# Two expert layers behind windowed attention: the output sums turned by VectorE in 32x32 blocks and stored in runs of 128 bytes, in place of TensorE's transposes

## What is computed

```python
w = softmax(weight_gen)                  # (2, 4096, 8 heads, 7 taps)
x = einsum('bshk,bskhg->bshg', w, x_unf) # 7 earlier tokens, 192 = 8 heads x 24
h = x @ w_in                             # 8192 x 192 by 192 x 2048
g = h * np.cos(h);  x = g @ w_out        # back to 192
h = x @ moe2_w_in
g = np.maximum(0.01 * h, h);  out = g @ moe2_w_out   # (8192, 192), float32
```

## Time and profile before

| | |
|---|---|
| median of 3 runs | 1163.77 us (1163.77 to 1166.3) |
| profiled execution | 1166.25 us |
| its span, first to last instruction | 1164.4 us |
| TensorE (PE) busy | 1146.1 us, 98% |
| VectorE (DVE) busy | 900.9 us, 77% |
| ScalarE (ACT) busy | 735.9 us, 63% |
| granted TensorE clock, mean | 0.997 |

### The profile page before, as it was taken

The page is one execution under the profiler, slowest core; times in us unless marked ns, Lnnn a source line. Parts: engine busy times, 40 slices in busy tenths (PEclk is TensorE's granted clock), DMA queues, the critical chain, the costliest instruction groups (busy, mean ns, idle before and its releaser), DMA issues.

```text
span 1164.4 us, 23292 instructions
## 1 busy us (share of the span) xinstructions
PE 1146.1 (98%) x10170; PEld 950.1 (82%) x10170; DVE 900.9 (77%) x862; ACT 735.9 (63%) x804; POOL 84.9 (7%) x81
## 2 busy tenths in 40 slices
PE   7889999999999999999999999999999999999998
PEld 5768888888888888888888888888888888888876
DVE  8878797878879788697786868868697886968433
ACT  5666674766657676575755747566575655757554
POOL 5850000000000000000000000000000000000000
PEclk9999999999999999999999999999999999999999
DMA  9760101001010000101001010000101001000000
GB/s 260 202 120 1 35 1 49 1 2 49 1 49 1 20 30 1 49 1 49 1 2 48 1 48 1 22 28 1 48 2 49 1 1 48 1 15 1 15 1 28
DMA packets 20653, 37.40 MB, mean 32 GB/s; under 512 B 5196, under 2 KB 14794, under 8 KB 20168
## 3 DMA queue, kind: packets, MB, share of 16 engines
q1 hardware_dynamic: 16104, 30.66, 8.4%
q0 software_dynamic: 4448, 5.24, 2.5%
HBM read 29.61 MB, written 6.29 MB: 31 GB/s over the span
## 4 chain that ended last, share of the span: by engine, by line
PE 92%; DVE 2%; SPq 2%; POOL 2%; ACT 1%; issue 1%; DMA 1%; ACTq 0%; POOLq 0%
PE slot L1064 43%; PE acc_a L1064 28%; PE acc_b L1064 19%; DMA x_win<-in_x 1%; DVE g_lo L825 1%; POOL prods L307 1%; POOL prods L298 1%; SPq L463 0%; DVE prods L307 0%; POOL out_hi_lo L554 0%; PE slot L1009 0%; DVE gate L897 0%; PE acc_b L1037 0%; PE slot L996 0%; ACT g_hi L637 0%
## 5 line engine op out<-in xcount | busy, mean ns | idle before, releaser
L1064 PE MATMUL acc_a<-g_hi,out_hi_lo 64*128 64x512 f32 x2000 | 697.5, 389 | 0.0
L1064 PEld LDWEIGHTS acc_a<-g_hi,out_hi_lo 64*128 64x128 f32 x2000 | 369.0, 184 | 36.8
L825 DVE TENSOR_TENSOR g_lo<-gate,g_hi 128x1024 fp32r<-128x1024 f32 x248 | 303.6, 1224 | 117.5 <-ACT g_hi L637 116.9
L1064 PE MATMUL acc_b<-g_hi,out_hi_lo 64*128 64x512 f32 x1000 | 389.1, 389 | 1.6 <-DVE g_lo L825 1.5
L1064 PE MATMUL acc_b<-g_lo,out_hi_lo 64*128 64x512 f32 x1000 | 387.5, 387 | 0.0
L1064 PE MATMUL acc_a<-g_lo,out_hi_lo 64*128 64x512 f32 x1000 | 387.3, 387 | 0.0
L637 ACT ACTIVATE g_hi<-gate 128x1024 fp32r<-128x1024 f32 x248 | 262.9, 1060 | 94.3 <-PE acc_b L1064 77.5
L1064 PE MATMUL slot<-x_a_hi,in_a_lo 64*128 64x512 f32 x1024 | 299.6, 394 | 5.2 <-DVE g_lo L825 2.5
L1064 PE MATMUL slot<-x_b,in_b_hi 64*128 64x512 f32 x1024 | 296.4, 388 | 0.2 <-DVE x_b L839 0.2
L1064 PE MATMUL slot<-x_a_lo,in_a_hi 64*128 64x512 f32 x1024 | 296.3, 387 | 0.0
L1064 PE MATMUL slot<-x_a_hi,in_a_hi 64*128 64x512 f32 x1024 | 296.2, 387 | 0.0
(11 more groups left out here) (100 smaller groups left out, 1073.9 us busy)
## 6 DMA issues: line engine op xcount, KB each, us to landing
x_win<-in_x SPq DMA_DIRECT2D x14, 960.0 KB, 4.7
out<-result SPq DMA_DIRECT2D x16, 384.0 KB, 2.3
out_raw<-in_moe_w_out SPq DMA_DIRECT2D x3, 512.0 KB, 8.5
out_hi_lo<-in_moe_w_out POOLq DMA_DIRECT2D x2, 768.0 KB, 11.0
out_hi_lo<-in_moe_w_out POOLq DMA_DIRECT2D x1, 1536.0 KB, 14.5
taps_w<-in_weight_gen SPq DMA_DIRECT2D x2, 560.0 KB, 9.4
in_a_raw<-in_moe_w_in SPq DMA_DIRECT2D x1, 1024.0 KB, 5.3
out_raw<-in_moe_w_out SPq DMA_DIRECT2D x1, 1024.0 KB, 11.6
```

The lines of the kernel that those rows point to most:

```text
L825: nc.vector.tensor_tensor(g_lo[:, q % 2, :], result_of(i - b, q), g_hi[:, q % 2, :].bitcast(FP32), ALU.subtract)\
L1064: return nc.tensor.matmul(to, w[rows, :], x[rows, :], start=start, stop=stop)
```

## The change

The output step of the first 15 chunks goes. In its place DVE, at step 14 of iteration i, turns `res_a` and `res_b` of chunk i-2 in blocks of 32x32 (`turn_result`), after the low part of step 12's unit. Within such a block tokens and channels have then changed places, but the blocks stand where they stood, so the stores gather them: 24 DMAs a chunk, each with 32 partitions x 4 runs of 32 values (128 bytes). The last chunk goes through TensorE as before.

```diff
-OUTPUT_STEP = 13
+TURN_STEP = 14
+BLOCK = 32
...
-        if step == OUTPUT_STEP:
-            return "output" if 2 <= i <= LAST else None
...
+                to = out_rows[:, c * row:(c + 1) * row]\
+                    .rearrange("(k t) (j d) -> t j k d", t=BLOCK, j=J)
+                sp.wait_ge(turned, 2 * c + 1)
+                for j in range(J):
+                    for d in range(0, DA, BLOCK):
+                        sp.dma_start(to[:, j, :, d:d + BLOCK],
+                                     turned_a[d:d + BLOCK, j * P:(j + 1) * P]
+                                     .rearrange("t (k d) -> t k d", d=BLOCK)).then_inc(stored, 16)
+                sp.wait_ge(turned, 2 * c + 2)
...
+            def turn_result(i):
+
+
+                c = i - 2
+                if c:
+                    dve.wait_ge(stored, 16 * STORES * c)
+                dve.wait_ge(acc_a_out, second_phase(i - 1) + 1)
+                nc.vector.transpose(turned_a[:, :], res_a[:, :]).then_inc(turned, 1)
+                dve.wait_ge(acc_b_out, second_phase(i - 1) + 1)
+                nc.vector.transpose(turned_b[:, :], res_b[:, :]).then_inc(turned, 1)
...
+                if step == TURN_STEP and i >= 2:
+                    turn_result(i)
...
-                if after == OUTPUT_STEP and kind(i, after) == "output":
-                    both_products(i, q, i, q - LAG, lambda: wait_for_output(i))
-                    transpose_output(slots[OUTPUT_STEP % SLOTS])
```

More of the change, by code:

```diff
@@ L208, in window_attention_two_ffn @@
         result = sb("result", [P, J, dim])
+        turned_a = sb("turned_a", [P, N])
+        turned_b = sb("turned_b", [P, N // 2])
         ident = sb("ident", [P, P])
@@ L266, in window_attention_two_ffn @@
         acc_b_out = sem("acc_b_out")
+        turned = sem("turned")
         result_ready = sem("result_ready")
@@ L435, in result_of @@
             return gate[:, q % 2, :]
+        STORES = J * dim // BLOCK
         block = ctx.enter_context(nc.Block())
@@ L496, in store, with store_last @@
             def store(c):
-                sp.wait_ge(result_ready, c + 1)
-                sp.dma_start(out_rows[:, c * row:(c + 1) * row],
+                to = out_rows[:, c * row:(c + 1) * row]\
[7 more added lines that the diff above has]
+                sp.wait_ge(turned, 2 * c + 2)
+                for j in range(J):
+                    for d in range(0, DB, BLOCK):
+                        s = j // 2 * DB + d
+                        sp.dma_start(to[:, j, :, DA + d:DA + d + BLOCK],
+                                     turned_b[s:s + BLOCK, j % 2 * P:(j % 2 + 1) * P]
+                                     .rearrange("t (k d) -> t k d", d=BLOCK)).then_inc(stored, 16)
+            def store_last():
+                sp.wait_ge(result_ready, 1)
+                sp.dma_start(out_rows[:, (C - 1) * row:],
                              result[:, :, :].rearrange("p t d -> p (t d)")).then_inc(stored, 16)
@@ L509, in _ @@
                 load_x(i + 2)
-            for c in range(C - 4, C):
+            for c in range(C - 4, C - 1):
                 store(c)
-            sp.wait_ge(stored, 16 * C)
+            store_last()
+            sp.wait_ge(stored, 16 * (STORES * (C - 1) + 1))
         @block.gpsimd
@@ L659, in leave_mid_a, with leave_res_a @@
                 nc.scalar.activation(mid_a[:, :], acc_a[:, :], ACT.Copy).then_inc(acc_a_out, 1)
-            def leave_res_a():
+            def leave_res_a(i):
+                if i >= 2:
+                    act.wait_ge(turned, 2 * (i - 1) - 1)
                 nc.scalar.activation(
@@ L666, in leave_res_a, with move_result @@
                     .then_inc(acc_a_out, 1)
-            def move_result(i, step, c):
+            def move_result(i, step):
                 act.wait_ge(filled, fills(i, step))
-                if c >= 1:
-                    act.wait_ge(stored, c * 16)
                 src = slots[step % SLOTS]
@@ L718, in step_of @@
                     split_second_high(i, step)
-                if kind(i, step) == "output":
-                    move_result(i, step, i - 2)
                 if step == INPUT_STEP - 1 and input_splits(i, INPUT_STEP):
@@ L749, in step_of @@
                     act.wait_ge(summed, unit(i - 1, 15) + 1)
-                    leave_res_a()
+                    leave_res_a(i - 1)
                 first_read(i, step)
@@ L803, in _ @@
             act.wait_ge(summed, unit(LAST, 15) + 1)
-            leave_res_a()
-            move_result(LAST, FINAL_STEP, C - 1)
+            leave_res_a(LAST)
+            move_result(LAST, FINAL_STEP)
         @block.vector
@@ L1158, in wait_for_slot @@
                     pe.wait_ge(leaky_ready, second_units(j, UNITS.index(s)))
-                elif what == "input":
+                else:
                     pe.wait_ge(x1_ready, j * 2 + 4)
-                else:
-                    pe.wait_ge(result_ready, j - 1)
             def wait_to_fill(i, q):
@@ L1233, in wait_for_input @@
                 pe.wait_ge(att, i * ATT_STEPS + 2 * ATT_STEPS)
[L1235 to L1238, removed]
             def rest_of_iteration(i, q):
                 after = UNITS[q] + 1
-                if after == OUTPUT_STEP and kind(i, after) == "output":
-                    both_products(i, q, i, q - LAG, lambda: wait_for_output(i))
-                    transpose_output(slots[OUTPUT_STEP % SLOTS])
-                elif after == INPUT_STEP and kind(i, after) == "input":
+                if after == INPUT_STEP and kind(i, after) == "input":
                     both_products(i, q, i, q - LAG, lambda: wait_for_input(i, INPUT_STEP))
```

## The result

| | before | changed |
|---|---|---|
| median, 5 runs each on one chip | 1165.18 us (1163.77 to 1166.3) | 1158.62 us (1158.38 to 1160.24) |
| profiled execution | 1166.25 us | 1158.45 us |
| its span | 1164.4 us | 1156.7 us |

The ratio is 0.9948, 95% interval 0.9937 to 0.9960: 6.1 us faster, where 6.3 were forecast. The forecast time, 1157.5 us, was reckoned from 1163.77, the median of the first three runs of the kernel before; five runs give 1165.18. The measured 1158.62 lies in the range, 1155.0 to 1161.3.

A forecast was written before the change was run, and what follows sets the result against it. TensorE, busy for 98% of the span, was taken to bound the kernel. Its 6.6 us gained less 0.3 us lost to the turn gave -6.3 us, from 1163.77 to 1157.5 us, range 1155.0 to 1161.3.

The forecast's parts named there:

- TensorE's 0.44 us a chunk: TensorE, border of steps 12 and 14: removing the output step shortens 1.35 us to 0.91, 15 times, 6.6 us gained.
- ScalarE's moves 0: ScalarE, two moves a chunk removed: it is idle 26 us in 70, so this gives TensorE nothing, 0.
- The turn at 1.1 us: VectorE, step 14: both transposes together take 0.68 + 0.42 us, read from rows of the same shapes.
- turn in iterations 3 and 5, 0.3 us: VectorE ahead of the input split: 1.1 us of transposes exceed 0.93 us idle, so 0.3 us lost in all.
- grows from 0.3 to 0.5 us: Sign in iterations 3 and 5: TensorE's wait for step 14's low part lengthens by that much.
- SP at 0.45 us an issue, hidden: SP's queue: 24 stores take 10.8 us a chunk beside TensorE's work, and cost 0, at the end too.
- One store after the other: Rival: stores land singly, 2.3 us each, 55 us a chunk, delaying loads; about 1340 us. Chance 0.02.
- The window's load: Load behind the stores in SP's queue: lands at 639.1, VectorE reads at 663.36, 24 us to spare, cost 0.
- The covers of 2.5 and 0.9 us: VectorE time that transposes at step 14 may take for nothing: 2.5 us in iterations 2 and 4, 0.93 in 3 and 5.
- That of 5.1 us: Ordinary iterations: 3.50 us idle ahead of the input split plus 1.57 us slack hide transposes up to this length.

The follow-up runs named there:

- act_moves: The changed kernel with ScalarE's two moves a chunk put back at step 13, results unread; ratio to before 0.9950.
- no_turn: The changed kernel without VectorE's transposes and small stores, sums stored untransposed with two DMAs a chunk, so output order is wrong; ratio to before 0.9951.
- step8: The changed kernel with VectorE's transposes at step 8 in place of 14; ratio to before 0.9952.
- sine15: The changed kernel with ScalarE's sine table reload in iterations 1, 3 and 5 at step 15 in place of 14, behind the input split; ratio to before 0.9933.
- stores2: The changed kernel with each small store cut in two, 48 DMAs of 128 runs of 64 bytes a chunk; ratio to before 1.0011.
- turn3: The changed kernel with each of VectorE's transposes made three times, 3.4 us a turn; ratio to before 1.0012.

## Why the prediction was right

- **TensorE's 0.44 us a chunk are the gain: shown.** TensorE's transposes back, gain gone; ScalarE's moves back, gain kept. The distance of starts was the right measure: the busy times of the two groups of transposes, 0.41 + 0.29 us, would have promised 10.5 us.
- **ScalarE's moves 0: shown** by act_moves.
- **The turn at 1.1 us: right**, 0.70 + 0.41. The Trainium skill's table ("VectorE: DVE Perf Modes", "The three transpose paths"), scaled by blocks, gave 1.87 us. Its 311 ns are for one tile of 128x128 of two-byte values; between 128x256 and 128x512 here lie 302 ns for 256 columns, which leaves some 0.1 us fixed in each instruction, and six tiles count it six times. That accounts for a part of the difference only. The measurement decides.
- **The term "turn in iterations 3 and 5, 0.3 us": the step that failed.** It was worked out from 1.1 us of turn against 0.93 us of idle time ahead of the split, and the turn causes no loss there: it fits, no_turn and step8 have the same hole without it, and sine15 closes the hole with the turn in its place. The sum went wrong one step earlier. It gives TensorE its 0.44 us in all 15 iterations, though it says itself that in 3 and 5 TensorE already waits for step 14's low part. An engine that waits for another gains nothing by arriving earlier. So nearly the whole 0.44 us was lost, twice. Around iteration 3 it is 0.18 us ahead of the input step (the next point but one) and 0.23 us behind it, where the low part comes when ScalarE's table load lets it; around iteration 5 it is 0.18 and 0.25 us. That makes 0.8 us in place of 0.3. (The 0.3 us of the earlier trace rows were no measure of the wait: from start to start the old hole was 0.07 us over a border without one.)
- **The total came nearer than its terms, and that is luck.** 0.5 us more were lost than forecast, and 0.3 us came back with the hole of iteration 6, which nobody had seen. The sign that was to show the turn, a wait that "grows from 0.3 to 0.5 us", came true (0.30 to 0.51) for another reason.
- **A second, smaller hole** in iteration 3 (starts at 264.97, 265.23, 265.54, some 0.1 us) stands where TensorE waits for attention's last sum, over at 265.08; the later reload leaves it as it is. It goes with the 0.18 us that the period which ends there lacks. That cause is read from the timeline and wasn't tried.
- **SP at 0.45 us an issue, hidden: right**, 0.48, and stores2 showed where the cover ends. The Trainium skill's rule that runs under 512 bytes miss line rate and bring a read-modify-write ("DMA: Bandwidth & Descriptors", "Specifications") may hold of the engines' bandwidth, and no run here shows such an operation; but 128 bytes cost 11.5 ns a packet and the queue that issues was the limit. The rule had no say in the time.
- **One store after the other: excluded**; a store landed in 1.5 us in the median (3.7 at most), and 24 were issued in 11.5.
- **The window's load: right**, landed 27 us ahead of its use, where 24 were read off.
- **The covers of 2.5 and 0.9 us**: turn3 met them with 6.3 us, the clock left out, for 6.6. That of 5.1 us is shown up to 3.4.

## What to carry to other kernels

When one engine paces a loop, cost a change by the distance of starts on that engine across the place, with and without; busy times of overlapped instructions promise more. Work for another engine is free as long as it fits the idle time ahead of its next wait plus the slack of the one who waits for it; the same 3.4 us cost 7.4 us, or nothing that could be told, by their place. And a faster pacing engine uses up slack of its neighbours: look for the iterations in which it waits for them already. There count no gain at all, and look for what makes them late; moving it may bring the gain back.

## What the runs showed of the hardware

- A float32 transpose in 32x32 blocks on VectorE, 128x512, takes 0.70 us, 128x256 0.40; a subtraction of 128x512 takes 0.68.
- A store of 128 runs of 128 bytes from 32 partitions is issued in 0.43 us in the median and lands in 1.5; runs of 64 bytes don't change the 0.47 us from one issue to the next. The engines took 11.5 ns a packet of the 128-byte runs.
- In turn3 a stall of TensorE of some 2.3 us in three pieces, the longest 1.2 us, behind a loop that had run at full clock for long, was followed by 3.4 us at the lower clock. A stall of the same pieces two iterations later was not.
- A load of ScalarE's table took 1.28 us, and work behind it in ScalarE's order came that much later (sine15).
